# A fused attention and mixture-of-experts kernel: attention's scores in quarters of TensorE, and placed behind the carried outputs

## The chip, the cores and the metric

The kernel runs on one core of a Trainium2 chip. The metric is device time in microseconds. The kernel before took 841.08 us, the median of three runs (840.84 to 841.57).

## The reference, cut to what matters

The reference chains three layers: a linear attention with a decaying state, a mixture of eight experts with a greedy routing by capacity, and a gated layer. Only the first is touched here. For 4 batches and 8 heads, 768 positions and a head width of 48 it computes

```
for t in range(S):
    state = alpha[:, :, t, :, None] * state + np.einsum('bhd,bhe->bhde', k[:, :, t], v[:, :, t])
    y[:, :, t] = np.einsum('bhd,bhde->bhe', q[:, :, t], state)
```

## The kernel before, in words

Attention works in chunks of 128 positions. There are 6 chunks and 4 batches, so 24 units; unit u is chunk u // 4 of batch u % 4. Eight heads of 48 rows are held as four pairs: heads of even number on partitions 0 to 47, those of odd number on 64 to 111, so a tile holds 128 partitions and 4 x 128 columns.

Inside a chunk the recurrence is written with products. A running product of alpha (`decay`) scales q to `q_dec`, and its inverse scales k to `k_und`. The scores of a chunk are k_und times q_dec (keys by queries), masked to be causal; the own outputs are v times the masked scores; the carried outputs are the state times q_dec; and the state is advanced by k times v.

Each engine runs its own program, and semaphores tie them. All orders are written out by hand. Chunk 0 is written out, chunks 1 to 4 are a loop over four unit steps, chunk 5 is written out again.

TensorE, one step of unit u (`step`, L441): `own_outputs` (L410) of u, which waits until the scores of u are masked; `update` (L431), which makes the addition to the state from `k_tok` and v; `carried_outputs` (L421), missing in chunk 0; `gate_and_turn` (L438) of unit u-1, which turns outputs to rows and makes the routing's logits; `keys_of` (L399), which transposes k_und of unit u+2; and `scores_of` (L385) of unit u+2. In chunk 5 there is no update and there are no keys, and scores only for the last two units.

VectorE, one iteration u: `decays` of u+2 (L199, a scan, and a reciprocal), `mask_scores` of u (L231), `advance` of u-1 (L245, adds to the state, waits for update and carried outputs of u-1), `undecays` of u+2 (a scan L214 and a product L224, whose end is the semaphore `k_ready`). Before the scan of unit n, `decays` waits for `ends_scaled` of unit n-4, since decay has four buffers.

ScalarE, one step of unit u (`step`, L343): state scaling of u-1 (L340), copy of the outputs' columns (L310), copy of rows (L318) and logits (L323) of u-1 after the turn, the store's DMA issue (L328), copy of turned keys of u+2 (L302), and the small copy of decay's ends of u (L333), which gives `ends_scaled`. Every second step also splits weights for the last layer (L1531).

GpSimd makes `q_dec` (L288, semaphore `q_ready`). SyncE issues the loads: q, k and alpha of unit u+5 once q and k of unit u+2 are done, and v for unit u+4 after update u.

A matmul of fp32 leaves two records each for the weight load and the matmul in the profile, so 8 matmuls show as x16; a transpose leaves one.

Of the kernel before, what the change touches and what calls it, by code (L numbers as in the profile page):

```python
# [18 lines left out]
P = 128  # L19
# [8 lines left out]
PAIRS = H // 2  # L28
HALF = 64
# [12 lines left out]
def attention(nc, qka, v, turn_gate, ident, causal, x_rows, stored, logits, w, quick, consts):  # L42
# [4 lines left out]
    with ExitStack() as ctx:  # L47
        def sb(name, shape, dt=F32):
            return ctx.enter_context(nc.sbuf_tensor(name, shape, dt))

        def ps(name):
            return ctx.enter_context(nc.psum_tensor(name, [P, 512], F32))

        def sem(name):
            return ctx.enter_context(nc.semaphore(name))
# [8 lines left out]
        k_und = [sb(f"k_und{r}", [P, PAIRS, SEG]) for r in range(2)]  # L64
# [15 lines left out]
        ps_scores = [[ps(f"ps_scores{i}{g}") for g in range(2)] for i in range(2)]  # L80
# [23 lines left out]
        masked = sem("masked")  # L104
# [17 lines left out]
        def unit(i, j):  # L122

            return B * i + j, j % B, i + j // B
# [246 lines left out]

        @block.tensor
        def _(pe):
            def scores_of(i, j, started=True):

                u, b, c = unit(i, j)
                if started:

                    pe.wait_ge(masked, u - 1)
                pe.wait_ge(q_ready, u + 1)  # L380
                pe.wait_ge(k_ready, u + 1)
                for a in range(PAIRS):
                    for g in range(2):
                        rows = slice(HALF * g, HALF * g + D)
                        mm = pe.matmul(ps_scores[j % 2][g][:, a * P:(a + 1) * P], k_und[j % 2][rows, PAIRS - 1 - a, 0:P],  # L385
                                       q_dec[b][rows, a, :], start=True, stop=True)
                mm.then_inc(scores_ready, 1)

            def keys_of(i, j, started=True):

                u, b, c = unit(i, j)
                pe.wait_ge(k_ready, u + 1)
                if j > 0 or started:

                    pe.wait_ge(k_tok_ready, u)
                else:
                    pe.wait_ge(idt_in, 16)
                for a in range(PAIRS):
                    tr = pe.transpose(ps_k[:, a * P:(a + 1) * P], k_und[j % 2][:, PAIRS - 1 - a, 0:P], idt[:, :])  # L399
                tr.then_inc(kt_ready, 1)  # L400

            def own_outputs(i, j, first_chunk=False):

                u, b, c = unit(i, j)
                pe.wait_ge(v_loaded[b], 16 * (c + 1))
                pe.wait_ge(masked, u + 1)
                for a in range(PAIRS):
                    for g in range(2):
                        h = 2 * a + g
                        mm = pe.matmul(ps_y_cols[HALF * g:HALF * g + D, a * P:(a + 1) * P], v_in[b][:, D * h:D * (h + 1)],  # L410
                                       scores[j % 2][:, h, :], start=(a == 0), stop=(first_chunk and a == PAIRS - 1))
                if first_chunk:
                    mm.then_inc(y_cols_ready, 1)

            def carried_outputs(i, j):

                u, b, c = unit(i, j)
                for a in range(PAIRS):
                    for g in range(2):
                        rows = slice(HALF * g, HALF * g + D)  # L420
                        mm = pe.matmul(ps_y_cols[rows, a * P:(a + 1) * P], state[b][rows, a, :],  # L421
                                       q_dec[b][rows, a, :], start=False, stop=(a == PAIRS - 1))
                mm.then_inc(y_cols_ready, 1)

            def update(i, j):

                u, b, c = unit(i, j)
                pe.wait_ge(k_tok_ready, u + 1)
                for a in range(PAIRS):
                    for g in range(2):  # L430
                        mm = pe.matmul(ps_state[HALF * g:HALF * (g + 1), a * D:(a + 1) * D],  # L431
                                       k_tok[j % 2][:, a, HALF * g:HALF * (g + 1)], v_in[b][:, D * (2 * a + g):D * (2 * a + g + 1)],
                                       start=True, stop=True)
                mm.then_inc(update_ready, 1)

            def gate_and_turn(i, j, into=y_turned_out):
                for a in range(PAIRS):
                    mm = pe.matmul(into[:, a, :], y_cols[j % 2][:, a * P:(a + 1) * P], turner[:, a, :],  # L438
                                   start=True, stop=True)
                mm.then_inc(y_turned, 1)  # L440

            def step(i, j, first=False, first_chunk=False, ahead=True, keys=True, updated=True, ends=False):
                u, b, c = unit(i, j)
                if not first:

                    pe.wait_ge(y_cols_copied, u)
                own_outputs(i, j, first_chunk)
                if not first_chunk:

                    pe.wait_ge(state_ready, u - 3)  # L450
                if updated:
                    if not first:

                        pe.wait_ge(state_added, u)
                    update(i, j)
                if not first_chunk:
                    carried_outputs(i, j)
                if ends:
                    pe.wait_ge(state_added, UNITS - B)
                    quick.turn_ends(pe)  # L460
                if not first:
                    if not (isinstance(u, int) and u == 1):

                        pe.wait_ge(lg_copied, u - 1)
                    else:
                        pe.wait_ge(turner_in, 16)
                    gate_and_turn(i, j - 1)
                if keys:
                    keys_of(i, j + 2)
                if ahead:  # L470
                    scores_of(i, j + 2)


            def fill(count):
                for n in range(count):
                    pe.matmul(ps_y_cols[:, 0:512], warm[:, 0, 0:P], warm, start=True, stop=True)

            def fill_wide(count, cols):
                for n in range(count):
                    pe.matmul(ps_y_cols[:, 0:cols], zeros[:, 0:P], zeros[:, 0:cols], start=True, stop=True)  # L480

            pe.wait_ge(zeroed, 2)
            fill(WARMUPS)
            for j in range(2):
                scores_of(0, j, started=False)
                keys_of(0, j, started=False)
                if j == 0:
                    pe.wait_ge(wide_zeroed, 1)
                    fill_wide(4, 512)
                    fill_wide(5, CAP)  # L490
                else:
                    fill(FILL[j])
            for j in range(B):
                step(0, j, first=(j == 0), first_chunk=True)
            with pe.Fori(1, CH - 1) as i:
                for j in range(B):
                    step(i, j)
            for j in range(B):
                step(CH - 1, j, ahead=(j < 2), keys=False, updated=False, ends=(j == B - 1))
            quick.spread_ends(pe)  # L500
            pe.wait_ge(y_cols_copied, UNITS)

            pe.wait_ge(k_tok_ready, UNITS - B + 2)
            gate_and_turn(CH - 1, B - 1, last_turned_out)
# [1625 lines left out]
```

## Time and profile before

| | before |
|---|---|
| median of 3 runs | 841.08 us |
| profiled execution, its own time | 841.45 us |
| its span | 839.5 us |
| TensorE busy | 811.9 us (97%) |
| VectorE busy | 505.7 us (60%) |
| ScalarE busy | 299.8 us (36%) |
| GpSimd busy | 242.9 us (29%) |
| granted TensorE clock, mean over the span | 0.983 |

The span is the time from the first to the last instruction of the profiled execution; the time of a run has some 2 us around it. Attention ends at about 131 us; routing follows, and then experts and the last layer, in which TensorE is busy nearly all of the time. A busy share over the whole span therefore says little on attention, and the stage is read by itself.

### The profile page before, as it was taken

Reading aid. Unit: us, or ns where it says so; the run is one execution under the profiler, and the core shown is the slowest. Engines: PE = TensorE matmul, PEld = TensorE weight load, DVE = VectorE, ACT = ScalarE, POOL = GpSimd, SP = SyncE. Lnnn points to the kernel's source line nnn. Section 1 sums busy time; section 2 is a strip of 40 time slices with the busy share of each in tenths; the row PEclk is TensorE's granted clock in tenths of the full one; section 3 lists DMA queues with packets and bytes.
Section 4 is the critical chain, followed back from the end, with each engine's and each line's share of the span. In section 5 each row is a group of like instructions: output and inputs, shape, how many; then the busy total and the mean of one; then the engine's idle time right before and its main releaser. Section 6 shows DMA issues by size and latency. Waiting matters only on the chain.

```text
span 839.5 us, 16444 instructions
## 1 busy us (share of the span) xinstructions
PE 811.9 (97%) x6005; PEld 776.7 (93%) x6005; DVE 505.7 (60%) x1134; ACT 299.8 (36%) x607; POOL 242.9 (29%) x276
## 2 busy tenths in 40 slices
PE   9999994899999999999999999999999999999995
PEld 5888883699999999999999999999999999999995
DVE  8999986847554755475546554655465546542332
ACT  2566652432343234322432333233323332333221
POOL 3322211488713041304130413050405040504001
PEclk9999996799999999999999999999999999999999
DMA  8898853402300230023002300230023002300000
GB/s 294 278 319 297 294 168 96 163 1 76 104 23 6 75 103 19 9 75 103 19 9 75 103 19 9 75 103 19 9 75 103 19 9 75 103 19 10 1 1 32
DMA packets 25777, 71.16 MB, mean 85 GB/s; under 512 B 3552, under 2 KB 10336, under 8 KB 25744
## 3 DMA queue, kind: packets, MB, share of 16 engines
q1 hardware_dynamic: 19152, 56.39, 20.6%
q0 software_dynamic: 3136, 9.64, 3.6%
q10 hardware_dynamic: 3456, 4.72, 1.5%
q8 instruction: 17, 0.28, 0.1%
q14 instruction: 16, 0.13, 0.1%
HBM read 61.30 MB, written 9.44 MB: 84 GB/s over the span
## 4 chain that ended last, share of the span: by engine, by line
PE 81%; DVE 2%; issue 1%; DMA 0%; POOLq 0%; ACT 0%; POOL 0%; DVEq 0%; ACTq 0%
PE ps_up L1919 48%; PE ps_acc L1919 30%; PE ps_turn_again L1128 1%; PE ps_turn L1925 1%; PE ps_turn_again L917 0%; DMA x_tok<-x_rows,slot_token 0%; DVE quick_at_row L831 0%; PE ps_turn_again L1154 0%; PE ps_up L1925 0%; DVE quick_at_row L980 0%; PE ps_up L2012 0%; POOLq L2051 0%; PE ps_acc L2017 0%; DVE quick_base L844 0%; DVE x_low L1903 0%
## 5 line engine op out<-in xcount | busy, mean ns | idle before, releaser
L1919 PE MATMUL ps_up<-z_high,gated_high 128*128 128x384 f32 x576 | 195.7, 340 | 0.0
L1919 PE MATMUL ps_up<-z_low,gated_high 128*128 128x384 f32 x576 | 192.8, 335 | 0.0
L1691 POOL TENSOR_TENSOR w_low<-w_raw,w_high 128x384 fp32r<-128x384 f32 x124 | 122.3, 1013 | 243.6 <-ACT w_high L1780 243.1
L1919 PE MATMUL ps_up<-z_high,gated_low 128*128 128x384 f32 x576 | 192.5, 334 | 0.0
L1919 PEld LDWEIGHTS ps_up<-z_high,gated_high 128*128 128x128 f32 x576 | 108.4, 188 | 0.0
L1919 PEld LDWEIGHTS ps_up<-z_high,gated_low 128*128 128x128 f32 x576 | 108.2, 188 | 0.0
L1919 PEld LDWEIGHTS ps_up<-z_low,gated_high 128*128 128x128 f32 x576 | 108.1, 188 | 0.2
L1864 DVE TENSOR_TENSOR act_out<-ps_up,act_out 128x384 f32<-128x384 f32 x96 | 53.4, 556 | 87.7 <-ACT act_out L1796 86.0
L1799 ACT CAST u_high<-ps_up 128x384 fp32r<-128x384 f32 x96 | 46.3, 482 | 167.8 <-DVE ps_up L1868 167.8
L1919 PE MATMUL ps_acc<-gated_high,u_high 128*128 128x384 f32 x288 | 96.9, 336 | 0.0
L1919 PE MATMUL ps_acc<-gated_high,u_low 128*128 128x384 f32 x288 | 96.5, 335 | 0.0
L1796 ACT ACTIVATE act_out<-ps_up 128x384 f32<-128x384 f32 x96 | 47.2, 492 | 137.7 <-PE ps_up L1919 137.6
L1919 PE MATMUL ps_acc<-gated_low,u_high 128*128 128x384 f32 x288 | 96.3, 334 | 0.0
L1714 POOL DMA_INDIRECT out<-o_tok,to_rows x24 | 23.7, 986 | 220.1 <-ACT o_tok L1808 185.2
L1871 DVE TENSOR_TENSOR u_low<-ps_up,u_high 128x384 fp32r<-128x384 f32 x96 | 53.5, 557 | 52.6 <-ACT u_high L1799 52.6
L1853 DVE SCALAR_TENSOR_TENSOR h_low<-ps_up,h_high 128x384 fp32r<-128x384 f32 x64 | 35.6, 557 | 68.7 <-ACT h_high L1776 66.7
L1868 DVE TENSOR_TENSOR ps_up<-act_out,ps_up 128x384 f32<-128x384 f32 x96 | 54.0, 563 | 37.1 <-PE ps_up L1919 34.8
L1780 ACT CAST w_high<-w_raw 128x768 fp32r<-128x768 f32 x64 | 53.7, 839 | 47.1 <-PE ps_acc L1919 35.4
L1919 PE MATMUL ps_up<-x_high,w_high 128*128 128x384 f32 x192 | 66.8, 348 | 0.1
L1919 PE MATMUL ps_acc<-h_high,w_high 128*128 128x384 f32 x192 | 64.8, 337 | 0.0
L1919 PE MATMUL ps_acc<-h_low,w_high 128*128 128x384 f32 x192 | 64.4, 336 | 0.2 <-DVE h_low L1853 0.2
L1919 PE MATMUL ps_up<-x_low,w_high 128*128 128x384 f32 x192 | 64.3, 335 | 0.0
(242 smaller groups left out, 1413.1 us busy)
## 6 DMA issues: line engine op xcount, KB each, us to landing
w_raw<-in_experts SPq DMA_DIRECT2D x64, 384.0 KB, 3.1
qka_in<-in_qka SPq DMA_DIRECT2D x22, 770.5 KB, 5.8
gated_raw<-in_gated SPq DMA_DIRECT2D x12, 576.0 KB, 5.8
v_in<-in_v SPq DMA_DIRECT2D x24, 192.0 KB, 5.6
x_rows<-y_rows ACTq DMA_DIRECT2D x24, 192.0 KB, 4.1
qka_in<-in_qka SPq DMA_DIRECT2D x2, 512.0 KB, 4.7
qka_in<-in_qka SPq DMA_DIRECT2D x2, 258.5 KB, 3.5
out<-o_tok,to_rows POOLq DMA_INDIRECT x24, 2.6
```

The lines of the kernel that those rows point to most:

```text
L1128: mm = pe.matmul(self.ps_count, self.at_row[:, j, :], self.slot_choice[:, j, :], start=(j == 0), stop=(j == SLOTS - 1))
L1691: part = pool.tensor_tensor(w.low[:, m % RING, cols], w.raw[:, m % RING, cols], w.high[:, m % RING, cols].bitcast(F32), ALU.subtract)
L1714: pool.indirect_dma_start(out=out, out_offset=bass.IndirectOffsetOnAxis(ap=to_rows[:, t:t + 1], axis=0), in_=o_tok[:, t, :], in_offset=Non ...
L1780: act.copy(w.high[:, m % RING, :], w.raw[:, m % RING, :]).then_inc(w_high_ready, 1)
L1796: act.activation(act_out[:, j % 2, :], ps_up[j % 2][0][:, 0:CAP], ACT.Sigmoid).then_inc(sigm_ready, 1)
L1799: act.copy(u_high[:, j % 2, :], ps_up[j % 2][0][:, 0:CAP]).then_inc(u_high_ready, 1)
L1853: dve.scalar_tensor_tensor(out=h_low[:, m % 2, :], in0=ps_up[m % 2][0][:, 0:CAP], scalar=0.0, in1=h_high[:, m % 2, :].bitcast(F32), op0=AL ...
L1864: dve.tensor_tensor(act_out[:, j % 2, :], ps_up[j % 2][0][:, 0:CAP], act_out[:, j % 2, :], ALU.mult).then_inc(silu_ready, 1)
L1868: dve.tensor_tensor(ps_up[j % 2][0][:, 0:CAP], act_out[:, j % 2, :], ps_up[j % 2][1][:, 0:CAP], ALU.mult).then_inc(gated_ready, 1)
L1871: dve.tensor_tensor(u_low[:, j % 2, :], ps_up[j % 2][0][:, 0:CAP], u_high[:, j % 2, :].bitcast(F32), ALU.subtract).then_inc(u_low_ready, 1)
L1919: mm = pe.matmul(acc, lhs[a], rhs[b], start=(first and i == 0), stop=(last and i == 2))
L1925: tr = pe.transpose(bank[:, t * P:(t + 1) * P], x_tok[:, t, k * P:(k + 1) * P], idt[:, :])
```

## The change

Three edits, all in TensorE's program of attention.

1. The scores of a head are made with two matmuls of 64 keys in place of one of 128. Which quarter of the array a matmul uses follows from the rows that it reads (head even or odd) and the output partitions that it writes (keys 0 to 63 or 64 to 127). The order over the quarters is (even, low), (odd, high), (even, high), (odd, low). There are 16 matmuls for a unit in place of 8, each with the same 128 columns of q_dec moved.
2. `scores_of` of unit u+2 moves from the end of a step to right behind the carried outputs of u, ahead of the turn of u-1 and the keys of u+2.
3. The waits for q and k of unit u+2 are taken out of `scores_of` and stand behind the own outputs, ahead of the waits for the state and ahead of `update`. A wait for `masked` that `scores_of` had is dropped.

```diff
-            def scores_of(i, j, started=True):
+            def wait_for_scores(i, j):
 
                 u, b, c = unit(i, j)
-                if started:
-
-                    pe.wait_ge(masked, u - 1)
                 pe.wait_ge(q_ready, u + 1)
                 pe.wait_ge(k_ready, u + 1)
+
+            def scores_of(i, j):
+
+                u, b, c = unit(i, j)
                 for a in range(PAIRS):
-                    for g in range(2):
+                    for g, h in ((0, 0), (1, 1), (0, 1), (1, 0)):
                         rows = slice(HALF * g, HALF * g + D)
-                        mm = pe.matmul(ps_scores[j % 2][g][:, a * P:(a + 1) * P], k_und[j % 2][rows, PAIRS - 1 - a, 0:P],
+                        keys = slice(HALF * h, HALF * (h + 1))
+                        mm = pe.matmul(ps_scores[j % 2][g][keys, a * P:(a + 1) * P], k_und[j % 2][rows, PAIRS - 1 - a, keys],
                                        q_dec[b][rows, a, :], start=True, stop=True)
                 mm.then_inc(scores_ready, 1)
...
                 own_outputs(i, j, first_chunk)
+                if ahead:
+                    wait_for_scores(i, j + 2)
                 if not first_chunk:
...
                 if not first_chunk:
                     carried_outputs(i, j)
+                if ahead:
+                    scores_of(i, j + 2)
                 if ends:
...
                 if keys:
                     keys_of(i, j + 2)
-                if ahead:
-                    scores_of(i, j + 2)
...
             for j in range(2):
-                scores_of(0, j, started=False)
+                wait_for_scores(0, j)
+                scores_of(0, j)
                 keys_of(0, j, started=False)
```

## Rows read from the trace of the kernel before

**Rows 1.** Stretches: us, busy of PE, PEld, DVE, ACT, POOL, clock, DMA share, GB/s
```profile
60.00:80.00 20.00, 20.00 (x303) 17.94 (x301) 18.48 (x29) 13.06 (x38) 4.73 (x4) 1.00 0.88 299
80.00:100.00 20.00, 20.00 (x302) 17.89 (x300) 18.46 (x29) 13.04 (x38) 4.72 (x4) 1.00 0.86 294
```
**Rows 2.** Timeline, TensorE, steady part: start us, length us, engine, line, operation
```profile
66.06 1.14 PE L438 MATMUL ps_y_rows<-turner,y_cols 128*128 128x104 f32 x8
...
67.57 1.16 PE L385 MATMUL ps_scores<-q_dec,k_und 48*128 48x128 f32 x16
...
68.66 1.08 PE L410 MATMUL ps_y_cols<-scores,v_in 128*48 128x128 f32 x16
...
69.57 0.62 PE L431 MATMUL ps_state<-v_in,k_tok 128*64 128x48 f32 x16
...
70.12 1.08 PE L421 MATMUL ps_y_cols<-q_dec,state 48*48 48x128 f32 x16
...
71.13 1.14 PE L438 MATMUL ps_y_rows<-turner,y_cols 128*128 128x104 f32 x8
...
72.10 0.60 PE L399 MATMUL ps_k<-quick_idt,k_und 128*128 128x128 f32 x4
```
**Rows 3.** Timeline, ScalarE and VectorE, steady part
```profile
67.29 0.48 ACT L318 COPY y_rows<-ps_y_rows 128x384 f32<-128x384 f32 x1 [0.47 <-PE ps_y_rows L438]
...
68.11 0.69 DVE L224 TENSOR_TENSOR k_und<-qka_in,k_und 128x512 f32<-128x512 f32 x1
...
68.87 0.21 ACT L333 ACTIVATE ends<-decay 128x4 f32<-128x4 f32 x1
...
69.12 1.23 DVE L199 TENSOR_TENSOR_SCAN decay<-qka_in,decay_starts 128x516 f32<-128x516 f32 x1 [0.31 <-ACT ends L333]
...
73.18 0.69 DVE L224 TENSOR_TENSOR k_und<-qka_in,k_und 128x512 f32<-128x512 f32 x1
```
**Rows 4.** Timeline, VectorE and TensorE, chunk 0 and its end
```profile
24.85 0.65 PE L431 MATMUL ps_state<-v_in,k_tok 128*64 128x48 f32 x16
...
25.26 0.69 DVE L224 TENSOR_TENSOR k_und<-qka_in,k_und 128x512 f32<-128x512 f32 x1
...
27.23 1.26 DVE L231 TENSOR_TENSOR scores<-ps_scores,mask 128x512 f32<-128x512 f32 x2
...
28.63 1.08 PE L410 MATMUL ps_y_cols<-scores,v_in 128*48 128x128 f32 x16 [0.53 <-DVE scores L231]
...
29.92 0.69 DVE L224 TENSOR_TENSOR k_und<-qka_in,k_und 128x512 f32<-128x512 f32 x1
...
34.11 0.62 PE L431 MATMUL ps_state<-v_in,k_tok 128*64 128x48 f32 x16
...
34.58 0.69 DVE L224 TENSOR_TENSOR k_und<-qka_in,k_und 128x512 f32<-128x512 f32 x1
```
**Rows 5.** Waits, 40 to 115 us: total us, times, longest us
```profile
DVE decay L199 <- ACT ends L333: 3.8, 12, 0.4
...
PEld ps_y_rows L438 <- issue: 2.8, 15, 0.2
PEld ps_scores L385 <- issue: 2.4, 14, 0.2
```
**Rows 6.** Timeline, TensorE, chunk 5
```profile
116.27 1.14 PE L438 MATMUL ps_y_rows<-turner,y_cols 128*128 128x104 f32 x8
...
118.43 1.08 PE L410 MATMUL ps_y_cols<-scores,v_in 128*48 128x128 f32 x16
...
122.61 1.08 PE L410 MATMUL ps_y_cols<-scores,v_in 128*48 128x128 f32 x16
...
129.09 1.14 PE L438 MATMUL ps_k<-turner,y_cols 128*128 128x104 f32 x8
```
**Rows 7.** One unit's carried outputs, whole and to 70.26: lengths ns, first and last start
```profile
L421 PE MATMUL ps_y_cols<-q_dec,state x16: 269/269/307, 70.1 to 70.9; 48*48 48x128 f32 x16
...
L421 PE MATMUL ps_y_cols<-q_dec,state x2: 307/307/307, 70.1 to 70.1; 48*48 48x128 f32 x2
```

## The prediction

> **What bounds the kernel now.** I read the stretches of the span first. Between 60 and 100 us of the run TensorE is busy for all 20 of every 20 us at a granted clock of 1.00, VectorE for 18.5 [rows 1]. The diff touches the attention stage alone, whose last matmul starts at 129.09 [rows 6]; the 710 us or so behind it are the same work before and after, so I read the stage unit by unit (24 units, 4 per chunk).
>
> In the timeline of TensorE [rows 2] one unit of the steady part is a closed sequence. From start to start: own outputs 0.91 (68.66 to 69.57), update 0.55, carried outputs 1.01, turn 0.97, keys 0.53, scores 1.09 (67.57 to 68.66). The sum is 5.06, and nothing stands idle except short changes of the array's shape. The list of waits names them: before the scores the weight loads stand still 14 times for 2.4 us, 0.17 each, and as long before the turn [rows 5]. So TensorE alone sets 5.06 us a unit.
>
> VectorE is close behind. In the first chunk, where carried outputs are missing, it is the one that sets the pace: its product into k_und starts at 25.26, 29.92 and 34.58, which is 4.66 apart [rows 4]. In the steady part it would still need 4.66, and stands idle for 0.31 before each new decay scan, released by ScalarE's small ends copy [rows 3, 5]. That wait matters below. It costs nothing today, because what VectorE delivers is early: the key product of 68.11 ends at 68.80, and its scores and keys are made at TensorE's 72.10 and later.
>
> **The change part by part.** Name u the unit of a step. A step now runs: own(u), wait for q and k of u+2, update(u), carried(u), scores(u+2), turn(u-1), keys(u+2).
>
> *Smaller matmuls.* Scores become 16 matmuls of 64 keys in place of 8 of 128, so 32 records in place of 16. What does a record cost? The carried outputs already run in quarters, on the two diagonal tiles: 16 records between 70.1 and 70.9, and two records start together at once, before any other is through [rows 7]. That is 8 pairs, some 0.108 us apart. If all four quarters work side by side as these two do, scores take 8 rounds of 0.108 = 0.87. This is the low bound: each tile has 8 records to stream whatever happens. The high bound is that no more than two ever work at once: 16 rounds of 0.108 = 1.73. In between, if weight loads for four tiles come no faster than they do for the update's two (64 columns, 16 records in 0.55, shape change included), 32 records take up to 1.10. I take 0.87: the nearest row is the carried outputs, the same tile size, the same 128 moved columns, and rows and columns of the array are each already shared by two (scores by rows, own outputs by columns, both paired).
>
> The Trainium skill speaks against this ("TensorE: Matmul & The Clock Gate", Part 3, The mechanism): matmuls start and end strictly in program order. Each fp32 matmul here leaves two records for the same tile, so by that rule the second one would hold back the next tile and only two tiles could overlap; the scores would be the 1.73. The trace bears the rule out in part only, since two records start together even at the very head of the carried outputs [rows 7], where strict order would show one alone. I keep it as a rival.
>
> *No shape change between carried outputs and scores*, both 64x64, and the scores' own disappears: 0.17 to 0.2 a unit. TensorE's own sum becomes 0.91 + 0.55 + 1.01 + 0.87 + 0.97 + 0.53 = 4.84 for a unit, 0.22 less than now. Were TensorE still alone in setting the pace, that would be the gain.
>
> *The order.* The wait for k and the work that feeds it move towards each other. The turn of u-1, the keys and all that hangs on them now come 0.87 later in the step, since scores stand ahead of them. And k of u+2, needed until now at the keys (3.44 after the start of own), is needed at the update (0.91 after it). Behind the waiting instruction stand update, carried, scores, turn and keys, so everything waits: VectorE's addition to the state (for update and carried), ScalarE's copies, SP's next v load. Is k late? Follow the loop that feeds it [rows 2, 3]:
> - turn(u-1) starts at 66.06. ScalarE copies y rows from 67.29, then logits, store issue, k_tok, and the ends copy at 68.87. The decay scan of u+4 starts at 69.12: 3.06 behind the turn. (k_tok doesn't wait for the keys: it starts 0.75 after they are done, behind ScalarE's own queue.)
> - VectorE runs scan, reciprocal, mask, state addition, scan, product: the product starts at 73.18 and ends at 73.87. That is 7.81 behind the turn, all of it VectorE's own work (mask and addition find their inputs ready).
> - From a VectorE end to the matmul it releases takes 0.14: mask 27.23 + 1.26 to own outputs at 28.63 [rows 4].
> - Then, new: update 0.55, carried 1.01, scores 0.87, and there stands turn(u+1).
>
> The loop is 7.81 + 0.14 + 0.55 + 1.01 + 0.87 = 10.38 for two units, 5.19 for one. Today the same loop has the k wait 2.5 us later in the step and no scores ahead of the turn, and is slack. Afterwards it is longer than TensorE's 4.84 and longer than the 5.06 of now. So the wait decides: +0.13 a unit against now, units alternating near 4.8 and 5.5 because the loop spans two.
>
> *How it begins.* In chunk 0 VectorE sets the pace and own outputs start straight behind the mask; the k product ends about 2 us behind it. The wait thus bites at once: update(2) moves from 24.85 to 25.26 + 0.69 + 0.14 = 26.09, and so on. In the first step with carried outputs, update(4) moves from 34.11 to 34.58 + 0.83 = 35.41, and turn(3) starts at 35.41 + 0.55 + 1.01 + 0.87 = 37.84. From there 16 turns, 8 rounds of the loop of 10.38, less one update that step 20 has not: turn(19) at 37.84 + 83.04 - 0.55 = 120.33. It is at 116.27 now [rows 6].
>
> *How it ends.* Of these 4.1 us, part is only order: behind turn(19) now come scores, own(21) starting at 118.43, 2.16 later. Afterwards own(21) follows directly, at 120.33 + 1.07 = 121.40, so 3.0 late. Step 21 waits once more for k(23). Turn(18) is one half round before turn(19); going up in pairs from turn(4) at about 42.8, I get 115.4, k(23) at the matmul at 123.35, while own(21) ends at 122.31: 1.0 lost; 0.87 of scores follow, where 1.07 stood, and one shape change less. Own(22) comes at about 126.3 in place of 122.61. Behind it nothing is changed: +3.7. An array that has been waiting starts its weight loads cold, 0.04 more at each of some 8 rounds: +0.3. Sum: +4.0 us.
>
> *Costed at nothing.* The wait on masked that is dropped was long fulfilled (own outputs wait for a later one). Waiting for q is covered by k, whose product ends 2 us later. Mask waits for scores less than now. SP's queue: the v load follows the update and the qka load the k product, both on a loop that is slower than now, at a DMA share of 0.88 [rows 1]; if TensorE did reach 4.84, the share would be 0.92, still no bound. PSUM banks and buffers are the same. Should these covers be gone, each is at most a few tenths a unit.
>
> The profiled execution took 841.45 for a span of 839.5, so it becomes 845.4; it lies 0.37 above the median of the three runs, 841.08, and against that the forecast is **845.1 us**.
>
> **The rivals.**
> *Only two tiles at once* (scores 1.73). TensorE's own sum is then 4.84 + 0.86 = 5.70, above the loop's 5.62, so +0.64 on 16 units, 10.2, and the same start and end as above with 0.86 more in each: about +14.5, 855.6. For it: no row shows more than two tiles busy. Against: rows and columns are each shared without loss today.
> *Weight loads bind a little* (scores 0.93 to 1.10): +4.3 to +6.5, 845.4 to 847.6. Inside my range.
> *The loop doesn't bind, TensorE does*: faster than before. The place is the k wait ahead of the update; it decides below 9.68 for the loop, 0.70 less than I count, for instance if ScalarE's ends copy came by that much earlier behind the turn. Then 16 units gain 0.22, 3.5 us, and the first chunk and the tail give nothing back: 837.6. For it: TensorE never idles now and VectorE's 4.66 allow 4.84. Against: every link of the loop is a row, and VectorE's part alone is 4.75 of it.
> *The change does nothing*: gain and loss cancel when the loop is near 10.1 for two units, 0.25 shorter than counted: 841.1.
>
> **How the numbers follow.** Chances: four tiles and the loop as counted, with small errors of the terms, 0.68; weight loads a little slower 0.09; two tiles at once 0.13; TensorE bound and faster 0.06; no difference 0.04. An error of 0.1 in the loop is 0.8 us over 8 rounds, and the start and end are good to a microsecond, so the likeliest case covers 843 to 847.5. With the slower weight loads and half of what lies between them and two tiles the range is 842.7 to 850.0. Two tiles at once and the faster rival stay outside. What counts as no change is 0.2%, 1.7 us. Faster 0.06, same 0.04, slower 0.90.
>
> **What would show it.** Four tiles: scores as 768 records, four starting within some 30 ns, and 0.87 us from their start to the turn's, without the shape change. The loop: TensorE idle before the update in every second unit or in all, released by VectorE's k_und product (L224), 0.3 to 0.7 each, and unit times alternating around a mean of 5.19. VectorE's idle before the decay scan grows from 0.31 to some 0.5, still released by ends. I am wrong if TensorE is busy throughout in the steady part (then look at its unit: 4.84 or 5.7), or if VectorE's part or ScalarE's between turn and scan has changed length.

## The result, and the profile after

The changed kernel takes 846.97 us (median of 4 runs, 846.38 to 847.07), the kernel before, timed beside it, 841.23 us (4 runs, 840.84 to 841.57). The ratio is 1.0066, with a 95% interval from 1.0054 to 1.0077: slower by 5.7 us. The forecast was 845.1 (842.7 to 850.0), slower.

The profiled execution took 846.91 us for a span of 845.1 us, 5.5 and 5.6 more than before. The stretches of the changed kernel, which answer to [rows 1] (columns as there), show where:

```profile
60.00:80.00 20.00, 18.68 (x352) 16.82 (x354) 17.54 (x27) 12.77 (x38) 4.31 (x4) 1.00 0.81 272
80.00:100.00 20.00, 18.69 (x346) 16.66 (x338) 17.60 (x26) 12.12 (x35) 3.97 (x4) 1.00 0.85 286
```

TensorE, busy for all 20 us before, now stands idle for 1.3 of every 20 at the same granted clock of 1.00, and VectorE has lost 0.9 of busy time: both wait for each other. The DMA share has fallen, from 0.88 and 0.86 in the two stretches to 0.81 and 0.85, and no engine waits for a transfer in the list that follows. The list of waits of the changed kernel from 40 to 115 us (total us, times, longest us), against [rows 5]:

```profile
DVE decay L199 <- ACT ends L333: 7.9, 7, 1.6
PEld ps_state L433 <- issue: 6.4, 7, 1.1
...
PEld ps_y_rows L440 <- issue: 2.4, 14, 0.2
PEld ps_y_cols L412 <- issue: 2.3, 14, 0.2
PE ps_state L433 <- DVE k_und L224: 2.1, 3, 0.7
```

The scores have no row any more, but their 2.4 us aren't gone: own outputs (ps_y_cols L412), which now follow the keys, have 2.3 us in 14 steps instead, so the idle behind the keys has only moved with the order (where the 0.22 us a unit does come from is told further down). New are the weight loads of the update (ps_state), which stand still for 6.4 us in 7 steps, and VectorE's idle before the decay scan has doubled, from 3.8 to 7.9. The view writes "issue" in four of TensorE's own waits for the update and names VectorE's k_und in three. The timeline shows that it is one cause. It holds four units of the steady part of the changed kernel; a number in brackets is idle time before the row and its releaser:

```profile
59.44 1.14 PE L440 MATMUL ps_y_rows<-turner,y_cols 128*128 128x104 f32 x8
...
62.63 1.23 DVE L199 TENSOR_TENSOR_SCAN decay<-qka_in,decay_starts 128x516 f32<-128x516 f32 x1 [1.18 <-ACT ends L333]
...
64.29 1.14 PE L440 MATMUL ps_y_rows<-turner,y_cols 128*128 128x104 f32 x8
...
66.69 0.69 DVE L224 TENSOR_TENSOR k_und<-qka_in,k_und 128x512 f32<-128x512 f32 x1
...
67.35 1.23 DVE L199 TENSOR_TENSOR_SCAN decay<-qka_in,decay_starts 128x516 f32<-128x516 f32 x1
67.48 0.67 PE L433 MATMUL ps_state<-v_in,k_tok 128*64 128x48 f32 x16 [0.61 <-issue]
68.08 0.97 PE L423 MATMUL ps_y_cols<-q_dec,state 48*48 48x128 f32 x14
...
69.96 1.14 PE L440 MATMUL ps_y_rows<-turner,y_cols 128*128 128x104 f32 x8
71.41 0.69 DVE L224 TENSOR_TENSOR k_und<-qka_in,k_und 128x512 f32<-128x512 f32 x1
71.47 1.08 PE L412 MATMUL ps_y_cols<-scores,v_in 128*48 128x128 f32 x16
72.38 0.62 PE L433 MATMUL ps_state<-v_in,k_tok 128*64 128x48 f32 x16
...
77.08 0.69 DVE L224 TENSOR_TENSOR k_und<-qka_in,k_und 128x512 f32<-128x512 f32 x1
78.11 0.67 PE L433 MATMUL ps_state<-v_in,k_tok 128*64 128x48 f32 x16 [0.72 <-DVE k_und L224]
78.72 0.97 PE L423 MATMUL ps_y_cols<-q_dec,state 48*48 48x128 f32 x14
...
80.60 1.14 PE L440 MATMUL ps_y_rows<-turner,y_cols 128*128 128x104 f32 x8
```

Read it from the product into k_und (L224) to the update behind it. The product of 66.69 ends at 67.38, the update starts at 67.48; the product of 77.08 ends at 77.77, the update starts at 78.11. The one between ends at 72.10, when own outputs (71.47 + 0.91 = 72.38) are still running, and holds nobody up. So every second step waits, and units alternate: from turn to turn 4.85, 5.67, 4.85, 5.79 (the turn not shown starts at 74.81). The mean is 5.29 against 5.06 before.

The way to +5.1 us at the last turn: turn(3) starts at 38.06 (35.67 before, +2.4), turn(19) at 122.05 (116.27 before, +5.8), own(22) at 127.70 (+5.1), the last turn at 134.19 (129.09 before, +5.1). The chunk 5 rows of the changed kernel, against [rows 6]:

```profile
122.05 1.14 PE L440 MATMUL ps_y_rows<-turner,y_cols 128*128 128x104 f32 x8
...
127.70 1.08 PE L412 MATMUL ps_y_cols<-scores,v_in 128*48 128x128 f32 x16
...
134.19 1.14 PE L440 MATMUL ps_k<-turner,y_cols 128*128 128x104 f32 x8
```

The half microsecond that is left of the 5.6 lies in the experts, which the diff doesn't touch: from the first expert matmul to the end of the span it is 682.5 us here and 681.9 before. One indirect store of outputs there starts after 3.67 us of waiting for an earlier one, at 762.70, where its like of before (756.50) had waited 2.44; that it makes the difference isn't shown. The same stretch lies between 681.9 and 682.5 in all the kernels that follow, so I count this as scatter.

### The profile page after: what moved, and what is told of

It reads as the page before. It is cut to its first block, busy times and chain, and to the rows that moved or that the text cites. A ratio compares the mean times of both kernels' runs of the same rounds, so it can differ in the third digit from the quotient of the medians.

```text
span 845.1 us, 17212 instructions
## 1 busy us (share of the span) xinstructions
PE 810.9 (96%) x6389; PEld 774.6 (92%) x6389; DVE 505.7 (60%) x1134; ACT 299.1 (35%) x607; POOL 243.0 (29%) x276
## 4 chain that ended last, share of the span: by engine, by line
PE 78%; DVE 2%; DMA 1%; issue 1%; POOL 0%; POOLq 0%; ACT 0%; DVEq 0%; ACTq 0%
PE ps_up L1924 47%; PE ps_acc L1924 29%; DMA out<-o_tok,to_rows 1%; PE ps_turn_again L1133 1%; PE ps_turn L1930 1%; PE ps_turn_again L922 0%; DMA x_tok<-x_rows,slot_token 0%; DVE quick_at_row L836 0%; PE ps_turn_again L1159 0%; PE ps_up L1930 0%; POOL w_low L1696 0%; DVE quick_at_row L985 0%; PE ps_up L2017 0%; POOL out L1719 0%; POOLq L2056 0%
```

## Experiments

Each of the eight kernels was run 5 to 11 times, beside the kernel before on the same chip; the times of before differ a little between rows for that reason. My theory: the smaller matmuls run on all four quarters of the array and, standing behind carried outputs, save a shape change (a gain); the early wait for k, with scores standing ahead of the turn, closes a ring through ScalarE and VectorE that is longer than TensorE's own unit (a larger loss). Rivals: the quarters themselves cost time (two at once only), or the new order costs it whatever the wait does.

| kernel | median us | before us | ratio (95% interval) | last turn at | steady unit |
|---|---|---|---|---|---|
| before | | | | 129.09 | 5.06 |
| changed | 846.97 | 841.23 | 1.0066 (1.0054 to 1.0077) | 134.19 | 4.85 / 5.7, mean 5.29 |
| quarters alone, old place (e1_quarters_only) | 840.75 | 841.19 | 0.9994 (0.9985 to 1.0003) | 128.57 | 5.01 |
| the wait late (e2_wait_late) | 838.35 | 841.19 | 0.9968 (0.9957 to 0.9979) | 125.39 | 4.85 |
| k wait last (e4_k_wait_last) | 846.07 | 841.19 | 1.0056 (1.0043 to 1.0070) | 133.35 | 4.85 / 5.6 |
| ends copy early (e5_ends_early) | 839.32 | 841.19 | 0.9979 (0.9970 to 0.9988) | 126.50 | 4.85 |
| 128 keys, changed order (e3_128_keys) | 848.78 | 841.39 | 1.0089 (1.0075 to 1.0103) | 136.56 | 5.07 / 5.7 |
| scores in old place (e7_old_order) | 842.30 | 841.39 | 1.0012 (1.0003 to 1.0021) | 129.55 | 5.01 |
| both cures (e6_late_and_ends_early) | 838.54 | 841.39 | 0.9965 (0.9952 to 0.9979) | 126.34 | 4.85 |
| late wait, 128 keys (e8_late_128_keys) | 841.63 | 841.18 | 1.0004 (0.9995 to 1.0013) | 129.37 | 5.07 |

### Quarters alone, in the old place

The kernel before, with its scores as 16 matmuls of 64 keys where they stood (and one long fulfilled wait ahead of them).

```diff
-                    for g in range(2):
+                    for g, h in ((0, 0), (1, 1), (0, 1), (1, 0)):
                         rows = slice(HALF * g, HALF * g + D)
+                        keys = slice(HALF * h, HALF * (h + 1))
 ...                      # the matmul takes 64 keys and writes 64 partitions
```

> The kernel before, with nothing but the scores' matmuls cut into quarters (16 of 64 keys), in their old place at the end of a step, their waits in front of them. If the loss comes from the order and the wait (my theory, the loop through ScalarE and VectorE), this one is neutral: 8 rounds of four tiles take 0.87 and the change of shape 0.2, together the 1.09 of now; 841.2 us, 840.5 to 841.8. If the quarters themselves cost (rival), it carries the loss of the changed kernel or much of it: 844 to 847.

Measured: 840.75 us, no difference that can be told from before. TensorE's timeline of this kernel:

```profile
67.73 1.10 PE L387 MATMUL ps_scores<-q_dec,k_und 48*64 48x128 f32 x32
68.76 1.08 PE L412 MATMUL ps_y_cols<-scores,v_in 128*48 128x128 f32 x16
```

32 records of scores in 68.76 - 67.73 = 1.03 us, where 16 larger ones took 1.09 [rows 2]. Two at once would have been 1.73 or more. The quarters cost nothing and bring 0.06 a unit. In this kernel's waits the weight loads stand still ahead of the scores as before (2.5 us over 15 steps) and now ahead of own outputs too (2.6 us over 15), so the 1.03 is some 0.87 of matmuls and 0.17 of standing still behind them. So the loss isn't the quarters'. (In the profiled execution one of VectorE's scans in chunk 0, at 23.96, took 1.73 us where it takes 1.22 elsewhere, and own outputs of unit 5 start 0.42 later than before; that is why 0.06 a unit shows as only 0.52 at the last turn.)

### The wait late

The changed kernel, with the waits for q and k moved from ahead of the update to right ahead of scores. An empty instruction (`nop`) stands between the waits and the first matmul of the scores; what it does by itself wasn't run.

```diff
-                if ahead:
-                    wait_for_scores(i, j + 2)
                 if not first_chunk:
 ...
                 if ahead:
+                    wait_for_scores(i, j + 2)
+                    pe.nop(nofuse=True)
                     scores_of(i, j + 2)
```

> The changed kernel, with the waits for q and k moved from ahead of the update to right ahead of the scores, behind the carried outputs. Loop theory: the wait then comes 1.6 us later in the step, the loop for two units falls from 10.6 to about 9.0, below TensorE's own 2 x 4.85; TensorE sets the pace at 4.85 a unit, 0.21 less than the kernel before, so 3.2 us over 15 units and 0.2 at start and end: 837.7 us, 837.0 to 838.6, faster than the kernel before. Rival, the waits cost by themselves (sequencer work, an array that starts cold) wherever they stand: 845 to 847. Rival, scores ahead of the turn cost by their order alone: 842 or more.

Measured: 838.35 us, faster than before by 2.8 us, and 8.6 less than the changed kernel, by the place of two waits. The stretch, the waits and the timeline of this kernel:

```profile
60.00:80.00 20.00, 20.00 (x394) 18.29 (x386) 19.32 (x31) 13.50 (x39) 5.02 (x5) 1.00 0.91 300
```
```profile
DVE decay L199 <- ACT ends L333: 0.6, 3, 0.2
```
```profile
62.15 1.08 PE L412 MATMUL ps_y_cols<-scores,v_in 128*48 128x128 f32 x16
63.02 0.69 DVE L224 TENSOR_TENSOR k_und<-qka_in,k_und 128x512 f32<-128x512 f32 x1
63.06 0.62 PE L433 MATMUL ps_state<-v_in,k_tok 128*64 128x48 f32 x16
...
64.32 0.33 PE L387 MATMUL ps_scores<-q_dec,k_und 48*64 48x128 f32 x2
...
65.50 1.14 PE L440 MATMUL ps_y_rows<-turner,y_cols 128*128 128x104 f32 x8
...
67.00 1.08 PE L412 MATMUL ps_y_cols<-scores,v_in 128*48 128x128 f32 x16
```

TensorE is busy throughout again, now at a unit of 4.85 (62.15 to 67.00). The k product ends at 63.71, 0.65 behind the update's start and 0.61 ahead of the scores: with the wait ahead of the update this very step would stand still; as it is, update and carried outputs cover it. The second rival, that the new order costs time by itself, falls. The DMA share of 0.91 is carried without a wait, as the 0.92 of the prediction was to be.

### The k wait last of the waits ahead of the update

The changed kernel; only the order of the waits differs, k's behind those for the state.

```diff
 own_outputs(i, j, first_chunk)
-if ahead:
-    wait_for_scores(i, j + 2)
 ...                      # the waits for state_ready and state_added
+    if ahead:
+        wait_for_scores(i, j + 2)
     update(i, j)
```

> The changed kernel, with the waits for q and k still ahead of the update but behind the two waits for the state, so that these are settled while TensorE stands. It takes the loop 0.34 us from the end of k's product to the update's first matmul now, where I had counted 0.14. If the difference is the sequencer's work on the waits behind k (theory), it falls to 0.14 to 0.24: 0.1 to 0.2 less for two units, 0.8 to 1.6 us over the stage: 845.4 to 846.2. If it is the semaphore and the array itself (rival), nothing changes: 847.

Measured: 846.07 us, 0.9 below the changed kernel. Its timeline:

```profile
66.35 0.69 DVE L224 TENSOR_TENSOR k_und<-qka_in,k_und 128x512 f32<-128x512 f32 x1
...
67.14 0.67 PE L433 MATMUL ps_state<-v_in,k_tok 128*64 128x48 f32 x16 [0.58 <-issue]
...
76.74 0.69 DVE L224 TENSOR_TENSOR k_und<-qka_in,k_und 128x512 f32<-128x512 f32 x1
77.53 0.67 PE L433 MATMUL ps_state<-v_in,k_tok 128*64 128x48 f32 x16 [0.47 <-issue]
```

An update of chunk 0 in the same kernel:

```profile
25.19 0.69 DVE L224 TENSOR_TENSOR k_und<-qka_in,k_und 128x512 f32<-128x512 f32 x1
...
26.19 0.67 PE L433 MATMUL ps_state<-v_in,k_tok 128*64 128x48 f32 x16 [0.49 <-DVE k_und L224]
```

From the product's end to the update is now 0.10 in both waiting steps (67.04 to 67.14, 77.43 to 77.53). In the changed kernel it was 0.10 in one and 0.34 in the other. That is 0.24 saved in every second waiting step, 4 in all: 1.0, and the last turn is 0.84 earlier.

The time came out as forecast, but the theory behind it, that the waits behind the released one cost the 0.24, isn't shown and doesn't fit all steps. In the changed kernel three waits stand behind k's in the loop (the two for the state, and that for k_tok in `update`), and it has 0.34 in units 4, 8, 12 and 16, the first step of each pass of the loop, and 0.10 in units 6, 10, 14 and 18, with the same waits. Here the wait for k_tok still stands behind k's, and while the loop has 0.10 throughout, units 2 and 3 of chunk 0 have 0.31 (25.88 to 26.19) and 0.26, where the changed kernel, with one wait more behind, has 0.10. So the number of waits behind doesn't set the gap; in each kernel it goes with the place in the program. It is on TensorE's side: SyncE's load of q, k and alpha, which waits for the same product, starts 0.07 behind its end in both kinds of step of the changed kernel (67.45 and 77.84). Its cause stays open.

### ScalarE's ends copy early

The changed kernel, its wait for k ahead of the update and all; on ScalarE the small ends copy, which releases the decay scan, goes ahead of the y rows copy.

```diff
 y_cols_copy(i, j)
+if to_scale:
+    end_scale(i, j)
 ...                      # y_copy, logits, the store's issue, k_tok
-if to_scale:
-    end_scale(i, j)
```

> The changed kernel, with ScalarE's small ends copy moved ahead of the rows' copy, so that VectorE's next decay scan no longer hangs on the turn. Loop theory: the loop is opened (it then runs from the carried outputs over the columns' copy, about 7.8 for two units), TensorE sets the pace at 4.85 a unit; the waits of chunk 0 still cost the 1.3 that own outputs of unit 5 are late: 841.2 + 1.3 - 15 x 0.2 = 839.5 us, 838.5 to 840.5. If the wait ahead of the update costs by itself, or something else feeds it late: 845 to 847.

Measured: 839.32 us, 7.7 below the changed kernel and faster than before. It cuts the ring, the loop of the prediction, at its other end. The timeline of this kernel:

```profile
61.84 0.21 ACT L333 ACTIVATE ends<-decay 128x4 f32<-128x4 f32 x1
62.11 1.14 PE L440 MATMUL ps_y_rows<-turner,y_cols 128*128 128x104 f32 x8
62.94 0.69 DVE L224 TENSOR_TENSOR k_und<-qka_in,k_und 128x512 f32<-128x512 f32 x1
...
63.55 1.23 DVE L199 TENSOR_TENSOR_SCAN decay<-qka_in,decay_starts 128x516 f32<-128x516 f32 x1
...
64.53 0.62 PE L433 MATMUL ps_state<-v_in,k_tok 128*64 128x48 f32 x16
```

The ends copy starts ahead of the turn that it used to follow by 2.8, and no row of this kernel's waits names it before the decay scan any more. The scan follows VectorE's own product, the k product ends at 63.63, 0.90 ahead of the update, and the unit is TensorE's 4.85. The last turn, 126.50, is 1.11 behind that of the late wait: this kernel still pays the wait in the first chunk.

### 128 keys in the changed order

The changed kernel with its scores as 8 matmuls of 128 keys.

```diff
-                    for g, h in ((0, 0), (1, 1), (0, 1), (1, 0)):
+                    for g in range(2):
                         rows = slice(HALF * g, HALF * g + D)
-                        keys = slice(HALF * h, HALF * (h + 1))
 ...                      # the matmul takes all 128 keys
```

> The changed kernel in its order and with its waits, but with scores of 128 keys, 8 matmuls, as before. The array then changes its shape between carried outputs and scores as well, so what stands between the start of the scores and the turn grows from 0.98 + 0.2 to some 1.3 or 1.4. Loop theory: that lies in the loop, 10.6 becomes 10.75 to 10.85 for two units, 1 to 2 us more over the stage: 848 to 849. If quarters bring nothing (rival): 847.

Measured: 848.78 us. In its waits the scores' weight loads stand still again (first fence), and scores take 65.32 - 64.23 = 1.09 from start to the turn's (second):

```profile
PEld ps_scores L386 <- issue: 2.6, 14, 0.2
```
```profile
64.23 1.16 PE L386 MATMUL ps_scores<-q_dec,k_und 48*128 48x128 f32 x16
65.32 1.14 PE L439 MATMUL ps_y_rows<-turner,y_cols 128*128 128x104 f32 x8
```

The ring turns in 10.74 (60.25 to 70.99) instead of 10.52 (59.44 to 69.96). The quarters make the changed kernel faster by 1.8 us (2.4 at the last turn); they aren't what slowed it.

### Scores back in their old place

The changed kernel, with scores behind turn and keys as before, their wait still ahead of the update.

```diff
 carried_outputs(i, j)
-if ahead:
-    scores_of(i, j + 2)
 ...                      # gate_and_turn, keys_of
+if ahead:
+    scores_of(i, j + 2)
```

> The changed kernel, with the scores put back to the end of the step, behind turn and keys, while the waits for q and k stay ahead of the update. Loop theory: the scores' 0.87 leave the loop, which is then about 9.7 for two units, below TensorE's 2 x 5.06, so the steady part is as before; what is left is the first chunk, where each update waits some 1.3 us for k: 842 to 844. Rival, an early wait costs the same wherever the scores stand: 846 to 847.

Measured: 842.30 us, 0.9 above before. The steady part never waits for k: the stretch from 60 to 80 us has TensorE busy for 20.00, at 5.01 a unit as with quarters alone. Without scores ahead of the turn the ring is 7.81 + 0.14 + 0.55 + 1.01 = 9.51, below two units of 5.01. What the early wait costs on its own is in the first chunk: own(5), the first that has carried outputs ahead of it, starts at 39.70 against 38.26. 1.44 lost there, some 17 units by 0.06 won back, 0.46 left at the last turn.

### Both cures

Late wait and early ends copy together (the two diffs above).

> Both repairs: waits right ahead of the scores, and ScalarE's ends copy ahead of the rows' copy. Loop theory: with the first alone TensorE already sets the pace, at 4.85 a unit, so the second adds nothing: 838.3 us, 837.6 to 838.9. If some of the wait for k is left in the first (rival), it takes up to 1 us more away: 837.3.

Measured: 838.54 us; by the ratios (0.9965 and 0.9968) it can't be told from the late wait alone. Its profile has one stall that the other doesn't, 1.2 us within one unit's keys:

```profile
43.58 0.55 PE L401 MATMUL ps_k<-quick_idt,k_und 128*128 128x128 f32 x3 [0.95 <-issue]
```

Nothing in the records releases it: it stands between two records of one group of transposes. Its cause stays open. But for it the last turn would be at some 125.2 (126.34 less the 1.17 by which that unit is longer than 4.85), 0.2 ahead of the late wait's.

### Late wait with 128 keys

The late wait's kernel with the scores' loop of before.

> The kernel with the late wait (waits right ahead of the scores, scores behind the carried outputs), but with scores of 128 keys in 8 matmuls. If the gain of that kernel over the one before comes from the shape change that goes between carried outputs and scores (theory), it is gone here, since 64x64 and 64x128 follow each other: TensorE's unit 5.06 or 5.07 again, 841.0 to 841.8 us. If it came from the order alone (rival), 838.4.

Measured: 841.63 us, the time of before. TensorE's timeline of this kernel:

```profile
66.20 1.16 PE L386 MATMUL ps_scores<-q_dec,k_und 48*128 48x128 f32 x16
67.30 1.14 PE L439 MATMUL ps_y_rows<-turner,y_cols 128*128 128x104 f32 x8
```

Scores take 1.10 here and 0.87 behind the same carried outputs when in quarters (5.07 a unit against 4.85). In the old place quarters brought 0.06 (5.07 to 5.01). So of the 0.22, some 0.16 come only with quarters and new place together. In this kernel's waits the weight loads stand still ahead of the scores again (2.8 us over 15 steps), where the late wait's kernel has no such row: quarters behind carried outputs, both 64x64, need no change of shape. Neither half of the change gives the whole gain alone.

## Why the prediction was right, and where it was 1.9 us short

**Four quarters at once: right.** From carried outputs' start to the turn I counted 1.01 + 0.87 = 1.88; it is 1.88 (62.41 to 64.29, 68.08 to 69.96, 78.72 to 80.60). The parts are cut otherwise than I wrote: scores start 0.70 behind the carried outputs and the turn 1.18 behind the scores, where my sign was 0.87. The records of one unit's scores (lengths in ns, first and last start), and the same unit in the timeline:

```profile
L387 PE MATMUL ps_scores<-q_dec,k_und x32: 268/269/321, 63.1 to 64.1; 48*64 48x128 f32 x32
```
```profile
63.11 0.33 PE L387 MATMUL ps_scores<-q_dec,k_und 48*64 48x128 f32 x2
63.21 0.28 PE L423 MATMUL ps_y_cols<-q_dec,state 48*48 48x128 f32 x2
63.27 1.09 PE L387 MATMUL ps_scores<-q_dec,k_und 48*64 48x128 f32 x30
```

32 records of 0.27 us start within 0.98 us, four every 0.109, where two at once would need 1.73. They even interleave: this unit's first two scores start at 63.11, the last two records of the carried outputs at 63.21. The rival of two tiles falls with this.

The rule that I had put beside it, "TensorE: Matmul & The Clock Gate" (Part 3, The mechanism) of the Trainium skill, has every matmul start in program order. Record by record the trace contradicts it. For whole matmuls it takes a step of working out, since the records at 63.21 may be the second ones of matmuls begun at 63.10: carried outputs keep the two diagonal tiles busy, with a record every 0.109 on each, so the scores of 63.11 must be on the other two tiles. Those are third and fourth in the program, ahead of the scores of the diagonal tiles, which can't start before carried outputs leave them.

**One shape change fewer: the size right, its place read wrongly.** TensorE's own unit was counted at 4.84 and is 4.85, in the steps that don't wait and in the late wait's kernel. But I said that the idle ahead of the scores goes (2.4 us in [rows 5]), and that is the change behind the keys, which is still there ahead of own outputs (2.3 us); from the keys' start to the start of what stands behind them it is 0.53 in both kernels. The change that is gone is the one between scores and own outputs. It was inside the 1.09 of the scores before, too short for the list of waits, and with quarters in the old place it shows there as own outputs' 2.6 us. The sum came out because it takes the whole 1.09 out and puts 0.87 in. "TensorEngine Tiling (Array Packing)" (Key Properties) of the Trainium skill says that the array drains when the tile mode changes; the trace agrees where the list of waits has a row, at some 0.17 a change, and carried outputs and scores, in the same mode, have none between them.

**The ring binds: right, by three cuts.** Moving the wait behind carried outputs, taking ScalarE's ends copy out of the ring, or taking scores out of it each ends the idling of the steady part; lengthening it by 0.2 (128 keys) lengthens the ring by 0.22. The part from the turn to the k product, 7.12, is as counted: 69.96 to 77.08. In the other kind of waiting step it is 7.25 (59.44 to 66.69), the 0.13 on ScalarE's side ahead of the scan. The trace of before had this too: from the turn at 55.93 to the product at 63.15 it is 7.22. I had read the link from one unit alone, the shorter kind.

**The term that was too small: the loop, above all the wake-up of the update.** I took 0.14 from the product's end to the update's first matmul, from the mask's release of own outputs [rows 4], and 0.55 for the update itself. It is 0.10 or 0.34, and the update takes 0.60 behind a wait: what I had called the cold array and put at 0.04 and outside the ring. Add both kinds up:
- 59.44 to 69.96: 7.25 + 0.69 + 0.10 + 0.60 + 1.88 = 10.52;
- 69.96 to 80.60: 7.12 + 0.69 + 0.34 + 0.61 + 1.88 = 10.64.

Their mean is 10.58 and I had 10.38. Of the 0.20 the gap is 0.08 in the mean, the update 0.05, and the last 0.07 is the longer way from turn to product in every second round. Over 8 rounds, of which the first took 10.75, that made turn(19) 1.5 later than forecast, besides 0.2 from the wake-up ahead of turn(3). I had given the loop an error of 0.1; it was 0.2. The k wait last gets 0.9 us of this back. The 0.14 was another matmul's: I had no row in which the update itself waits.

**Start and end.** Update(4) was forecast at 35.41 and came at 35.58, turn(3) at 37.84 and 38.06, in these rows of the changed kernel:

```profile
34.55 0.69 DVE L224 TENSOR_TENSOR k_und<-qka_in,k_und 128x512 f32<-128x512 f32 x1
...
35.58 0.67 PE L433 MATMUL ps_state<-v_in,k_tok 128*64 128x48 f32 x16 [0.68 <-DVE k_und L224]
...
38.06 1.14 PE L440 MATMUL ps_y_rows<-turner,y_cols 128*128 128x104 f32 x8
```

From turn(19) to own(22) I had 6.0 and it took 5.65: the last wait, in step 21, cost 0.6 (own at 123.12, carried outputs at 124.75, 1.63 between them against 1.01 before) and not 1.0. The sum over all terms: 0.2 + 1.5 - 0.35, less the 0.3 that I had added for the cold array, is 1.1 more than the 4.0 forecast, and 5.1 is what the last turn shows. The other 0.4 to 0.8 is the scatter of the experts and of the medians.

**The rivals.** Two tiles at once (855.6) and weight loads that bind (0.93 to 1.10 for the scores) fall with the 0.87 measured. "TensorE binds" (837.6) did not happen in the changed kernel, but it is what each cut of the ring turns it into: 838.35 and 839.32.

**Costed at nothing: right.** q, masked, SP's queue and the banks show up in none of TensorE's waits of the changed kernel. With TensorE at 4.85 VectorE is busy for 19.3 of 20 us at the late wait, so the next 0.2 a unit would have to come from it as well.

## What to carry to other kernels

Where buffers go round between engines, an engine that is busy all the time says nothing of how far the ring behind it is from binding: walk it from one matmul through ScalarE and VectorE back to the same matmul, over as many units as it spans, and compare with that many units of the busy engine. Here it spans two: decay has four buffers, and k is made two units ahead. Each thing put between the wait and the ring's start enters it, here scores ahead of the turn. Read each link from all kinds of unit in the loop, not from one. Alone neither they (the late wait) nor the early wait (scores in their old place) slowed the steady part, together they made it 5.29 a unit from 5.06. Put a wait right ahead of the instruction that needs it: the two lines moved (and an empty instruction behind them) are the difference between 846.97 and 838.35 us, the best version found.

Smaller matmuls paid here where they made neighbours alike in shape (0.22 a unit), and hardly by themselves (0.06). And for an instruction that will now really wait, count the wake-up and the first cold instruction inside the loop, at 0.1 to 0.35 and 0.05 here.

## What the hardware showed

- Four 64x64 tiles of the array stream at once in fp32 (32 records of 0.27 us start within 0.98 us), and matmuls of two different lines overlap on it: carried outputs' last records start 0.1 us after scores' first.
- Two diagonal tiles of the carried outputs, and the four of the scores in pairs, write into the same PSUM tile in different partitions at the same time, and each tile still takes a record every 0.109 us.
- The same release of TensorE costs 0.10 us in one step of the loop and 0.34 in another, by the step's place in the program; another order of the waits moves the longer gap to other steps (0.10 in the loop, 0.26 and 0.31 in chunk 0). Why is open.
- A stall of about 1 us between records of one group, released by nothing in the profile, appears once in the kernel with both cures (at 43.58 us) and in no other kernel's waits from 40 to 115 us.
